# A three-stage layer in one kernel: order of the sums, of the last expert tile and of the work between the halves

## What is computed

```
x = attn(q, k, v, w_phi)                 # 4x8 heads, 576 tokens, 64 wide -> 2304 x 512
e = argmax(x @ w_gate)                   # one of 8 experts per token
h = relu(x[e] @ w1[e]); y = gate * sigmoid(x @ w_og)[e] * (h @ w2[e])
a = y @ w_in                             # up half: 512 -> 2048
out = (a * sigmoid(a)) @ w_out           # down half: 2048 -> 512
```

## Time and profile before

| | us |
|---|---|
| median of three runs | 923.31 |
| lowest, highest | 922.99, 924.96 |
| the profiled execution | 921.94 |
| its span | 919.9 |
| PE busy | 887.3 |
| DVE busy | 552.2 |
| ACT busy | 430.3 |
| POOL busy | 297.5 |

### The profile page before, as it was taken

How to read it: one execution, slowest core, us unless ns; L and a number is a source line. 1 busy time by engine, 2 the same in 40 slices (tenths; PEclk the granted TensorE clock), 3 DMA queues, 4 the chain that set the end, 5 groups by cost and what they waited for, 6 DMA issues and landing times.

```text
span 919.9 us, 18945 instructions
## 1 busy us (share of the span) xinstructions
PE 887.3 (96%) x6841; PEld 793.2 (86%) x6842; DVE 552.2 (60%) x822; ACT 430.3 (47%) x794; POOL 297.5 (32%) x264
## 2 busy tenths in 40 slices
PE   7999999979999998999999999999999999999996
PEld 6888888868888887888888789999999999999996
DVE  4667777769503699920460065632668877777774
ACT  4555655543333433334444467655667533333331
POOL 4686776633534563554443200000000011111112
PEclk9999999989999999999999999999999999999999
DMA  5455555417512578461111046655377534334321
GB/s 154 139 151 153 152 151 154 119 38 258 189 46 84 175 244 273 159 171 46 57 46 35 24 118 181 178 148 136 95 209 200 168 117 115 117 128 124 116 92 46
DMA packets 129700, 122.00 MB, mean 133 GB/s; under 512 B 38064, under 2 KB 104752, under 8 KB 129648
## 3 DMA queue, kind: packets, MB, share of 16 engines
q1 hardware_dynamic: 122000, 103.10, 38.5%
q0 software_dynamic: 3440, 11.27, 3.8%
q10 hardware_dynamic: 4208, 6.93, 2.0%
HBM read 86.39 MB, written 34.88 MB: 132 GB/s over the span
## 4 chain that ended last, share of the span: by engine, by line
PE 65%; DVE 18%; issue 6%; SPq 4%; ACT 4%; DMA 1%; DVEq 0%; POOL 0%; ACTq 0%; POOLq 0%
PE bank L712 15%; PE bank L714 15%; PE bank L713 15%; DVE ops L1639 5%; PE bank L786 4%; PE bank L726 3%; PE bank L740 3%; DVE place L1639 3%; DVE w_raw L1540 2%; PE bank L913 2%; ACT ops L1266 2%; PE bank L707 2%; DVE w_hi L1511 2%; PE bank L767 1%; DVE tail L1540 1%
## 5 line engine op out<-in xcount | busy, mean ns | idle before, releaser
L695 POOL DMA_INDIRECT out<-temps,ids x18 | 25.1, 1394 | 345.1 <-DVE temps L1540 342.3
L669 POOL TENSOR_TENSOR h_lo<-h_raw,h_hi 128x512 fp32r<-128x512 f32 x49 | 73.1, 1513 | 155.9 <-ACT h_hi L1157 155.9
L712 PE MATMUL bank<-ops,place 128*128 128x384 f32 (+1 forms) x357 | 119.9, 336 | 2.8 <-ACT temps L1235 1.6
L714 PE MATMUL bank<-ops,place 128*128 128x384 f32 (+1 forms) x357 | 118.3, 331 | 0.0
L713 PE MATMUL bank<-ops,place 128*128 128x384 f32 (+1 forms) x357 | 118.3, 331 | 0.0
L712 PE MATMUL bank<-place,ops 128*128 128x256 f32 x294 | 84.8, 289 | 3.2 <-DVE ops L1639 2.7
L1602 DVE TENSOR_TENSOR temps<-temps,bank 128x384 f32<-128x384 f32 x72 | 39.7, 553 | 76.3 <-PE bank L714 76.1
L713 PE MATMUL bank<-place,ops 128*128 128x256 f32 x294 | 83.1, 283 | 0.0
L714 PE MATMUL bank<-place,ops 128*128 128x256 f32 x294 | 83.1, 283 | 0.0
L1511 DVE CAST w_hi<-ahead 128x1024 fp32r<-128x1024 f32 x48 | 48.5, 1010 | 55.7 <-PE bank L714 55.6
L712 PE MATMUL bank<-w_hi,h_hi 128*128 x200 | 80.3, 402 | 1.4 <-DVE h_lo L1575 1.3
(11 more groups left out here) (238 smaller groups left out, 2168.0 us busy)
## 6 DMA issues: line engine op xcount, KB each, us to landing
ahead<-in_moe_w SPq DMA_DIRECT2D x56, 512.0 KB, 4.7
h_rows<-temps SPq DMA_DIRECT2D x96, 192.0 KB, 2.5
w_raw<-h_rows SPq DMA_DIRECT2D x17, 512.0 KB, 4.1
y_sorted<-y ACTq DMA_DIRECT2D x25, 256.5 KB, 3.0
raw<-h_rows SPq DMA_DIRECT2D x10, 512.0 KB, 4.0
tail<-h_rows SPq DMA_DIRECT2D x9, 512.0 KB, 3.8
qk<-in_k SPq DMA_DIRECT2D x32, 128.0 KB, 2.6
vs<-in_v SPq DMA_DIRECT2D x32, 128.0 KB, 2.3
```

The lines of the kernel that those rows point to most:

```text
L669: nc.gpsimd.tensor_tensor(h_lo[:, fs, :], h_raw[:, fs, :], h_hi[:, fs, :].bitcast(F32), ALU.subtract).then_inc(h_lo_done, 1)
L712: mm(o, left_hi, right_hi, start=first, stop=False, skip_group_check=shared)
L714: return mm(o, left_lo, right_hi, start=False, stop=last, skip_group_check=shared)
```

## The change

Four things are moved. No product, cast or sum is added or taken away.

1. Down half. DVE makes the sums of granule g+4 where it made those of g+3, those of granule 3 once more in iteration 0. In the last granule PE goes product by product through both column blocks, not block by block.
2. Last expert tile. The first five y groups and the transposes of the first half of tile 24 are made inside tile 23 (first_groups before its tile_down, the transposes in its middle), the other transposes and three groups right after it; tile_down of tile 24 then runs in one piece. ACT follows: it moves the first groups before it stores tile 23, and stores tile 24 in step 0 behind the copies of M1, M5 and M6. DVE makes the low part of M5 and that of the last tile earlier. M2 of step 0 now waits for y of tile 23, M2 of step 1 for tile 24.
3. Between the halves. Granules 0 to 2 are loaded and summed one step earlier. The high and low part of granule 0 go from step 23 to the end of step 22 (on ACT behind silu of C22, in front of silu of C12). The low part of job 9 and the sums of job 11 go behind step 23, the two parts of job 11 into iteration 1.
4. The waits of slab 0 for weights stand only in front of the first product of a column block.

```
-            GRANULE_AT = {18: 0, 19: 1, 20: 2}
+            GRANULE_AT = {17: 0, 18: 1, 19: 2}
...
             def first_groups():
-                pe.wait_ge(y_moved, T_MAX - 1)
+                pe.wait_ge(y_moved, T_MAX - 2)
                 for k in range(5):
                     y_group(0, k)
-            def other_groups():
+            def last_tile():
+                hidden_transpose(T_MAX - 1, (1,))
                 for k in range(5, 8):
                     y_group(0, k)
+                e = expert_of(T_MAX - 1)
+                pe.wait_ge(split_half[1], (e + 1) * HALF)
+                tile_down(T_MAX - 1, 0, e % 2)
...
-            tile(T_MAX - 2, 1, load=False)
-            tile(T_MAX - 1, 0, up=False, load=False, beside=first_groups, between=other_groups)
+            tile(T_MAX - 2, 1, load=False, beside=first_groups, between=lambda: hidden_transpose(T_MAX - 1, (0,)))
+            last_tile()
...
-                    elif i == M2 and n == 1:
-                        pe.wait_ge(y_moved, T_MAX)
+                    elif i == M2:
+                        pe.wait_ge(y_moved, T_MAX - 1 + n)
...
-                for fp in range(2):
+                order = [(fp, m) for fp in range(2) for m in range(7)]
+                if g == GRANULES - 1:
+                    order = [(fp, m) for m in range(7) for fp in range(2)]
+                for fp, m in order:
...
-                    if s == 0:
+                    if s == 0 and m == D_M1:
                         pe.wait_ge(job_lo, NF - U_EARLY + f + 1)
...
-                if n == STEPS - 1:
-                    granule_high(0)
                 copy_out(n, M5, copy5, ps_c, copied5, C22)
                 copy_out(n, M6, copy2, ps_a, copied2, C12)
+                if n == 0:
+                    store_tile(T_MAX - 1, 0)
...
                 if n == STEPS - 1:
                     granule_high(1)
+                if n == STEPS - 2:
+                    granule_high(0)
                 silu(n, C12, copy2, v12_done)
...
-                elif STEPS - NF < n < STEPS - 1:
+                elif STEPS - NF < n < STEPS - 2:
                     job_low(n - (STEPS - NF) - 1 + NF - U_EARLY)
                 if 1 <= n < 5:
                     job_sums(n - 1)
-                elif n >= STEPS - NF:
+                elif STEPS - NF <= n < STEPS - 1:
                     job_sums(n - (STEPS - NF) + NF - U_EARLY)
-                if 20 <= n < 23:
-                    granule_sums(n - 20)
+                if 19 <= n < 22:
+                    granule_sums(n - 19)
+                if n == STEPS - 2:
+                    granule_low(0)
+            job_low(JOBS - 3)
             granule_low(1)
...
                 if g == 0:
+                    granule_sums(3)
+                    job_sums(JOBS - 1)
+                if g == 1:
                     job_low(JOBS - 1)
-                if g + 3 < GRANULES:
-                    granule_sums(g + 3)
+                if g + 4 < GRANULES:
+                    granule_sums(g + 4)
```

More of the change, by code:

```diff
@@ L904, in tile_up, with hidden_transpose @@
                 last.then_inc(h_done, 1)
-            def hidden_transpose(t):
-                for half in range(2):
+            def hidden_transpose(t, halves=(0, 1)):
+                for half in halves:
                     pe.wait_ge(h_moved, 2 * t + 1 + half)
@@ L1215, in _ @@
             nc.scalar.activation(stage[:, 1, CW - 1:CW], ident[:, 0:1], ACT.Silu)
-            tile(T_MAX - 2, 1, rows_too=False)
-            hidden_T(T_MAX - 1, 0)
-            hidden_T(T_MAX - 1, 1)
+            hidden_T(T_MAX - 2, 0)
+            hidden_T(T_MAX - 2, 1)
+            hidden(T_MAX - 1, 0)
+            hidden(T_MAX - 1, 1)
             for k in range(4):
@@ L1222, in _ @@
             op_high(0, M5)
[L1223 removed]
+            move_raw(0, 4)
+            hidden_T(T_MAX - 1, 0)
+            hidden_T(T_MAX - 1, 1)
+            store_tile(T_MAX - 2, 1)
+            for k in range(5, 8):
                 move_raw(0, k)
[L1225 to L1228 removed]
+            for i in (M6, M2, M7):
+                op_high(0, i)
             def copy_out(n, i, to, at, done, c):
```

52 lines of the change are left out of this document (24 added, 28 removed).

## The result

The changed kernel takes **911.72 us** (median of 4 runs, 909.18 to 915.67), the kernel before beside it 924.13 (4 runs): ratio 0.987, 95% interval 0.9832 to 0.9909. That is 12.4 us less, between 8.4 and 15.5 by the interval. The forecast was 912.1.

A forecast was written before the change was run, and what follows sets the result against it. PE had most to do, paced in the down half by a DVE-ACT ring. 12.5 + 3.3 - 4.0 - 1.7 - 0.2 + 1.3 = 11.2 us off 923.3 gave 912.1; 8 in 10 for 905.8 to 914.0.

The forecast's parts named there:

- pace of the down half: Down half: with sums two ahead PE sets the pace, 5.03 us a granule instead of 5.465; gain 13.7 us.
- late granule 3: Start of the down half: granule 3's load lands late and PE waits, 0.7 to 1.9 us in sum, taken as 1.2.
- clock fall behind it: Half clock after a PE wait: none forecast at granule 3; behind the step 2 wait, 1.7 us of work lost.
- wait in step 2: Step 2 of the up half: PE idles 4.0 us for ACT's copy of M1, ACT being held by step 0's stores.
- step 23: Between the halves: an old PE wait of 0.91 us goes, a new one of 1.2 comes; net -0.2.
- The ring: Down half: sums, high part, low part, sums across DVE and ACT take 5.33 us, longer than PE's 5.03 a granule.
- Part 3: Moved store of tile 24: step 0's stores land later, PE idles 4.0 us in step 2, half clock costs 1.7.
- part 1: Down half, sums two granules ahead: gain 13.7 us less 1.2 at the start, 12.5 us.
- A: Rival, step 2: the clock does not fall behind the wait; 910.4 us, chance 0.20.
- B: Rival: step 0's stores land 2.5 us after issue, so no wait or clock fall in step 2; 906.4 us, chance 0.13.
- C: Rival, down half: DVE stays in a ring with ACT; 918 us at half the gain, 924.6 at none; chance 0.11.
- D: Rival, down half: an unlanded load stops sums and low part; slower, about 926 at 13.2 us landing; 0.03 with the like.

The follow-up runs named there:

- e1: The kernel before with only DVE's sums made two granules ahead in the down half; 908.38 us, ratio 0.9841.
- e2: The kernel before with only the last tile's new order and the moved store of tile 24; 922.79 us, ratio 1.0013.
- e8: The changed kernel with granule 4's load ahead of step 23's stores and sums of granule 4 and job 11 ahead of granule 3's; 911.23 us (one run).
- e4: The kernel before with only the last granule done product by product; 920.55 us, ratio 0.9977.
- e9: The changed kernel with job 11's two loads behind step 23's four stores in SP's queue; 910.3 us (one run).
- e3: The changed kernel with step 0's four stores issued by SP ahead of the loads of jobs 0 and 1 and the row numbers; 906.75 us.
- the two mended wholes: e3 with the old order between the halves and granule 0's low part behind two additions, 903.08 us; e3 with e9's edit and high part back in step 23, 903.58.
- e7: e8 plus e3's edit and granule 0's high part back in step 23; 909.6 us, ratio 0.986.

## Why the forecast was right, and where it was not

The time, 912.1 against 911.72, is right, and closer than its working deserves: part of it is luck. Step by step, in the profiled execution:

| step | forecast | measured | by |
|---|---|---|---|
| pace of the down half | 13.7 | 13.4 | e1 |
| late granule 3 | -1.2 | -2.2 | after |
| clock fall behind it | none | -1.6 | after, e1 |
| last tile | 3.3 | 3.3 | e2 (1.4 + 1.9) |
| wait in step 2 | -4.0 | -3.6 | after |
| clock fall behind it | -1.7 | -1.6 | after, e8 |
| step 23 | -0.2 | -0.1 | after |
| last granule | 1.3 | 1.1 | e4 |
| sum | 11.2 | 8.7 | (8.9 from the table) |

**What held.** The mechanism of each part, with its place. The ring that paced the down half was read right, and so was the cover behind it: 28 granules at 5.04, casts released by PE. Part 3 was the risky step, a chain of five links from a moved store to PE two steps later, and each link came out within 0.5 us. Inside one of them two errors cancel: the last store was issued 8.5 us after the burst's start and not 7.1, because SP was held longer, and then took 2.8 to land and not 4.0. Its lesson is that the chain was found by asking, for a store that moves, what is queued behind it on every queue. The earlier trace rows already showed the fragile piece: stores that took 4.0 us behind a burst, and a silu that waited 0.63 for one.

**What failed.** The term "it lands 3.5 (alone, as here) to 4.3 us later" for the load of granule 3. The rows it came from the earlier trace rows show that load behind stores of which the last had gone 3.4 us before, and the forecast moved DVE's instructions without following what they release. The change puts the low part of job 9 behind step 23; job 11's load waits for it; SP, waiting for that, holds step 23's four stores; and these then stand right in front of the load of granule 3 (5.23 us). e9 undoes just this, and the load lands after 3.54 with the wait at 0.4: exactly the early end of the forecast (9.1 after the start of the down half, 0.4 late). The same question that found part 3's cost was not asked in part 1. With it, the term would have been about 2 (an estimate, from the landing of 5.23), and the second fall of the clock a risk of its own.

**How a sum that is 2.3 too high met the median.** The sum's base, a profiled execution 1.4 below the median of before, and the 8.9 of the trace would give 914.4. The median is 2.7 lower. The four runs spread over 6.5 us, and the untouched first 500 us alone vary by several; whether both clock falls came in each of the other three runs is not recorded, and e8 and the wait at 348 us show that they need not: without them the same kernel would gain 8.9 + 1.6 + 1.2 to 1.6, 11.7 to 12.1 (an estimate). The interval of the measured ratio (8.4 to 15.5 us) holds the one sum and the other. This much stays open.

**The rivals.** A, no fall of the clock in step 2, did not come in this execution, but it did not fall in e8, which has the same code there: 0.20 was not too much. B is refuted: behind the same loads the last of step 0's stores landed 11.3 us after the burst's start (551.29 + 2.83 - 542.83) and not 6.8, and with the loads behind the stores the wait is gone (e3). C and D did not occur: once the lead is there, DVE waits for a load once, 0.17 us. D's mechanism, a load that holds the sums and so all behind them, did appear at granule 3 for once, where no lead had been built.

## What to carry to other kernels

A reordering on one engine is also one on the queue that issues its DMAs: for each instruction that moves, ask which buffer its end sets free, which load waits for that, and which stores stand behind that load in the same queue. Both large losses here (5.3 us in step 2, 2.9 at granule 3) were of that kind, and both were mended by putting stores that somebody waits for, or that only need to be gone, ahead of loads that nobody needs yet, without touching the order on any engine. Build such a change from parts and run each alone: one of a few lines gave more than all together, one was worth nothing, and the two mended wholes (903.08 and 903.58 us) are 8 us better than the change as it came.

## What the runs showed of the hardware

- A store of 192 KB behind four loads of 256 KB and the row numbers on the same queue held the queue's issuer for 3.2 to 4.7 us in all twelve traces, against a median of 0.47 for SP's issues, and itself landed after 5.3 to 6.7. Step 0's stores, with the loads behind them, landed after 2.3 to 3.4.
- A load of 512 KB, the one of granule 3, landed 3.5 to 3.8 us after its issue when the last of four stores of 192 KB had been issued 3.4 to 3.9 us before it (before, e1, e9; in e9 two loads of 256 KB stood between), 5.2 when 1.1 before (after), and 5.9 when 1.4 before with one more load ahead of them (e7). The one edit of e9 took it from 5.23 to 3.54: the landing time went with what was issued just ahead on the queue.
- PE's granted clock fell to half behind a wait of 2.2 us and stayed full behind one of 3.4, in two kernels of nearly the same code. Behind one wait of the same instructions, 2.8 to 3.1 us from start to start, it fell in seven traces of twelve.
- The first 500 us, in which no kernel differs, took from 502.7 to 510.5 us. Below 1%, kernels are to be compared from a common landmark in their traces, and with the falls of the clock counted apart.
